# Second MLP of a fused attention and two-MLP kernel: one chunk in eight instead of one in four keeps its second product in fp32

## The reference

```
def _moe2_ref(x, w_in, w_out):
    h = x @ w_in            # 128 -> 2048
    g = h * np.cos(h)
    return (g @ w_out).astype(np.float32)   # 2048 -> 128
```

## Time and profile before

| what | value |
| --- | --- |
| median of 3 runs | 2633.49 us (2632.07 to 2635.88) |
| profiled execution | 2632.91 us |
| its span, first to last instruction | 2631.1 us |
| mean granted TensorE clock | 0.989 of full speed |
| busy over the span: PE, ACT, DVE, POOL | 98%, 92%, 89%, 78% |
| DMA | 17 GB/s mean |

### The profile page before, as it was taken

How to read it: one execution, slowest core, us unless ns; L and a number is a source line. 1 busy time by engine, 2 the same in 40 slices (tenths; PEclk the granted TensorE clock), 3 DMA queues, 4 the chain that set the end, 5 groups by cost and what they waited for, 6 DMA issues and landing times.

```text
span 2631.1 us, 38615 instructions
## 1 busy us (share of the span) xinstructions
PE 2584.3 (98%) x10691; PEld 1794.6 (68%) x10691; DVE 2341.6 (89%) x2730; ACT 2423.3 (92%) x3173; POOL 2052.3 (78%) x1474
## 2 busy tenths in 40 slices
PE   8699999999999999999999999999999999999999
PEld 5366656665666666665656688888888888888887
DVE  4599999999999999999999888888888888888887
ACT  5499999999999999999999899999999999999998
POOL 0189999999999999999999777777777777777776
PEclk9699999999999999999999999999999999999999
DMA  7000000000002000000000000000000000000000
GB/s 220 21 8 11 10 8 11 7 11 7 11 17 71 8 11 7 11 8 11 7 11 5 1 12 12 12 11 11 11 11 11 11 11 11 11 11 11 11 11 15
DMA packets 25688, 45.52 MB, mean 17 GB/s; under 512 B 2888, under 2 KB 11880, under 8 KB 25384
## 3 DMA queue, kind: packets, MB, share of 16 engines
q1 hardware_dynamic: 25640, 44.92, 5.7%
HBM read 16.99 MB, written 12.78 MB: 11 GB/s over the span
## 4 chain that ended last, share of the span: by engine, by line
PE 62%; POOL 14%; issue 10%; DVE 8%; ACT 4%; DMA 1%; POOLq 1%; DVEq 0%; ACTq 0%; SPq 0%
PE bank L1166 22%; PE bank L1158 20%; POOL work L379 8%; PE bank L1016 8%; PE bank L1023 8%; DVE work L776 5%; POOL work L367 3%; POOL part_hi L389 2%; ACT work L532 2%; DVE bank L758 1%; PE bank L947 1%; PE bank L1149 1%; ACT work L520 1%; POOL part_hi L383 1%; DVE work L767 1%
## 5 line engine op out<-in xcount | busy, mean ns | idle before, releaser
L446 POOL TENSOR_TENSOR act_lo<-work,act_hi 128x960 fp32r<-128x960 f32 (+1 forms) x416 | 723.4, 1744 | 330.1 <-ACT act_hi L607 322.1
L1023 PE MATMUL bank<-work,v 128*128 128x480 f32 x1664 | 742.5, 568 | 0.2 <-ACT tokens_t L539 0.2
L1016 PE MATMUL bank<-part_hi,stack_now 96*128 96x480 f32 x2496 | 665.0, 400 | 13.7 <-DVE stack_next L704 7.1
L379 POOL TENSOR_TENSOR work<-work 128x960 f32<-128x960 f32 x278 | 621.9, 2237 | 42.3 <-POOL work L367 3.4
L912 DVE SCALAR_TENSOR_TENSOR work<-work,bank 128x960 f32<-128x960 int32 x416 | 479.6, 1153 | 155.3 <-ACT work L594 155.3
L1016 PEld LDWEIGHTS bank<-part_hi,stack_now 96*128 96x128 f32 x2496 | 434.9, 189 | 241.8 <-DVE work L776 161.9
L758 DVE SCALAR_TENSOR_TENSOR bank<-bank,over_c,work 128x960 f32<-128x960 f32 x416 | 508.4, 1222 | 42.8 <-PE bank L1016 34.1
L776 DVE SCALAR_TENSOR_TENSOR work<-bank,coef_a,work 128x960 f32<-128x960 f32 x416 | 502.2, 1207 | 0.2 <-PE bank L1016 0.2
L515 ACT ACTIVATE work<-work,made 128x960 f32<-128x960 f32 x416 | 469.1, 1128 | 26.2 <-POOL work L379 26.2
L594 ACT ACTIVATE work<-bank 128x960 int32<-128x960 f32 x416 | 404.2, 972 | 93.1 <-PE bank L1158 93.1
L918 DVE TENSOR_TENSOR work<-work,bank 128x960 f32<-128x960 f32 x416 | 477.2, 1147 | 0.0
(11 more groups left out here) (120 smaller groups left out, 3039.3 us busy)
## 6 DMA issues: line engine op xcount, KB each, us to landing
x_group<-tokens_t SPq DMA_DIRECT2D x52, 240.0 KB, 2.2
out_dram<-work SPq DMA_DIRECT2D x52, 240.0 KB, 2.4
x_ring<-in_x_dram SPq DMA_DIRECT2D x40, 240.0 KB, 6.1
work<-in_x_dram SPq DMA_DIRECT2D x12, 240.0 KB, 4.0
stack_now<-stack_next SPq DMA_DIRECT2D x8, 288.0 KB, 3.0
work<-in_moe_w_in_dram SPq DMA_DIRECT2D x1, 1024.0 KB, 15.4
w_raw<-in_moe_w_in_dram SPq DMA_DIRECT2D x1, 1024.0 KB, 4.9
v<-in_moe_w_out_dram SPq DMA_DIRECT2D x2, 0.5 KB, 13.9
```

The lines of the kernel that those rows point to most:

```text
L379: nc.gpsimd.tensor_tensor(quot[k % 3], square[k % 3], abs_h[k % 3], ALU.add).then_inc(den_ready, 1)
L446: nc.gpsimd.tensor_tensor(act2_lo[:, k % 2, w], angle[k % ANGLES][:, w], act2_hi[:, k % 2, w].bitcast(F32), ALU.subtract).then_inc(act2_pa ...
L1016: mm = pe.matmul(place_out[:, t, :], stack_now[:, i, w], part_hi[0:K3, place, :], start=start, stop=stop, skip_group_check=not start)
L1023: mm = pe.matmul(sums, v[:, 2 * u + t, :], g[:, t * GROUP:(t + 1) * GROUP], start=(2 * u + t == 0), stop=(2 * u + t == CHUNKS - 1))
```

## The change

`split_to` gives 480 columns only to every fourth unit (units 3 and 7 of a group) instead of every second (1, 3, 5 and 7). So in units 1 and 5 of each group, 104 units in all, the second chunk goes in parts as well. `part_v2` parts four chunks instead of three for even j, since chunks 3 and 11 are now needed in parts; chunks 7 and 15 stay in fp32.

```diff
         def split_to(k):
 
-            return GROUP if k % 2 else UNIT
+            return GROUP if k % 4 == 3 else UNIT
...
             def part_v2(j):
 
-                c = slice(4 * j, 4 * j + 3)
+                c = slice(4 * j, 4 * j + (4 if j % 2 == 0 else 3))
                 nc.gpsimd.tensor_copy(v2_hi[:, c, :], v2[:, c, :]).then_inc(v2_parted, 1)
                 pool.wait_ge(v2_parted, 2 * j + 1)
                 nc.gpsimd.tensor_tensor(v2_lo[:, c, :], v2[:, c, :], v2_hi[:, c, :].bitcast(F32), ALU.subtract).then_inc(v2_parted, 1)
```

## The result

The changed kernel takes 2636.6 us (median of 20 runs, 2632.87 to 2639.82). The kernel before, run 20 times as well, takes 2631.47 us (2627.01 to 2635.88). The ratio is 1.0021, 95% interval 1.0014 to 1.0027: slower by 5.1 us, at the very edge of what the prediction called no change. The three runs known before it (2633.49) lay 2 us high, so the forecast time of 2636.0 is closer to the measured one than the forecast effect, +2.5 us, is to +5.1: that the times agree to 0.6 us is in part luck.

What follows compares the result with a forecast made beforehand. TensorE was taken to bound the kernel. Per group, 0.30 us saved against a 0.35 us stall behind GpSimd gave 0.05 us longer; 50 groups made 2.5 us, ScalarE and ends nothing: 2636.0 us, 8-in-10 range 2624 to 2646.

Steps and rivals of the forecast that it cites:

- What bounds: From 1700 to 2600 us TensorE is busy throughout and sets the time; no other engine does.
- Rival (d): The fp32 product is hidden, so the change does not do what it says; answered no, no chance stated.
- TensorE's saving: Second products of units 1 and 5: 0.15 us saved per changed unit, 0.30 a group, 15.6 us in all.
- ScalarE at nothing: High parts of units 1 and 5 take 0.40 us more each, covered by wait and spare time, costed at nothing.
- Rival (c): ScalarE becomes second late engine over three full units in a row: 5 us on top, 2641 us; chance 0.15.
- GpSimd: Longer low part of unit 1 delays `low_y` and unit 2's low part; TensorE waits in `end2(2)`, 0.35 us a group.
- The release: From the start of a 960-column low part to TensorE's next work behind its two matmuls: 2.83 us.
- The stall: TensorE's wait in `end2(2)` for unit 2's low part: next first product at 2003.90 instead of 2003.55, 0.35 us.
- The restart: TensorE resuming after the wait for GpSimd: 0.15 us of release and restart, stall bounds 0.20 and 0.54.
- The ends: First and last group, including `part_v2` and the end chain on GpSimd: cancel to within 0.3 us, taken as 0.
- (a): TensorE's gain stays because the low part of unit 2 isn't late: 2618 us; chance 0.15, whole or in half.
- (b): Slower: costlier restart in `end2(2)`; with the full weight load stall 0.54, 12 us, 2646 us; chance 0.2.

Runs made afterwards that it cites:

- run 20: Not a label of a follow-up: the kernel before was run 20 times, like the changed kernel; median 2631.47 us.
- TensorE's part alone: Against the changed kernel, ScalarE and GpSimd keep 480 columns in odd units, TensorE still does six float32r matmuls in units 1 and 5: 2614.2 us, ratio 0.9939.
- unit 1 alone: Against the kernel before, the change made only in unit 1 of each group, unit 5 keeping its fp32 product: 2644.05 us, ratio 1.0055.
- `low_y` elsewhere: The changed kernel with `low_y` issued one step later on GpSimd, behind the low part of unit 2: 2615.05 us, ratio 0.9944 to the kernel before.
- the widened side engines: Against the kernel before, ScalarE and GpSimd make 960 columns in units 1 and 5, TensorE keeps the fp32 product: 2646.98 us, ratio 1.0065.

## Why the prediction was right, and where it was off

What bounds: right. TensorE before; TensorE's part alone shows that taking work off it alone gives all of it back as time. Rival (d) falls with it.

TensorE's saving: 0.15 us a unit forecast, 0.158 to 0.160 measured in two kernels. Four passes at the distance of the float32r matmuls (the Trainium skill, FP8 and Floating Point Precision, TensorE Precision Notes) would have made it 0.21; the measurement decides for the rows.

ScalarE at nothing: right. After, its turns wait 200 times for TensorE, up to 0.3 us each, and the waits for line 918 stay at 8. At the place where the prediction counted on 0.04 us to spare, the high part of unit 1 and the turns of unit 4 now stand like this:

```profile
1995.61 0.99 ACT L607 CAST act_hi<-work 128x960 fp32r<-128x960 f32 x1
1996.57 0.98 ACT L594 ACTIVATE work<-bank 128x960 int32<-128x960 f32 x1
```

That is 0.96 us from start to start, where it was 0.93 before (1996.30 to 1997.23): the cover held to 0.03 us. Rival (c) is out for this change: neither the change in unit 5 alone nor the kernel with fp32 in units 1 and 7 loses anything.

GpSimd: the place, the mechanism and its count (once a group, 50 times) were right, each term a little small. Start to start of a full low part in this place is 2.24 us, not the 2.20 of rows 5, where the next step was the short cast and not `low_y`. The release is 2.85, not 2.83. The stall is 0.40 us in the group shown and 0.43 on the mean (3.03 less 2.60), and the lengths of the group give 0.118 + 2 x 0.159 = 0.44, against 0.35 forecast; in unit 1 alone 0.295 + 0.158 = 0.45. This is the term that was mis-sized, by 0.08 to 0.09 us. The terms above account for 0.06 of it; where the rest comes from is open. Since the net is a difference of two like numbers, 0.44 - 0.32 instead of 0.35 - 0.30, it doubled the effect: 0.118 us a group for 0.05, 5.1 us for 2.5. The point from which the prediction called it slower, 5.3 us, lies between the 5.9 us that the groups give and the 5.1 us of the times.

The restart: between the bounds of the prediction, 0.20 and 0.54, and at the row taken. The load and the matmul are again at the same moment, 2002.73, and the two matmuls take 0.53 us to the next work instead of 0.43. That a matmul can begin before its weight load completes is what the Trainium skill says (TensorE: Matmul & The Clock Gate, Architectural detail); the trace, with both at one start, does not speak against that. It does speak against what the prediction made of it, a restart that costs nothing: 0.1 us is lost, and no run here shows to what.

The ends: taken as 0. The second MLP begins at 1479.81 us in the trace of before and at 1477.23 in that of after, and lasts 1151.3 and 1157.0 us: 5.7 us more, where 50 groups of 0.118 are 5.9. In the last group TensorE now waits twice for low parts, 1.08 and 0.64 us, where it waited once:

```profile
2624.76 0.70 PE L1166 MATMUL bank<-act_lo,v_hi 128*128 128x480 f32 x2 [1.08 <-POOL act_lo L446]
...
2626.96 0.70 PE L1166 MATMUL bank<-act_lo,v_hi 128*128 128x480 f32 x2 [0.64 <-POOL act_lo L446]
```

Of the rivals (a) is what the kernel does with `low_y` elsewhere, 2615.05 us for the 2618 forecast. (b) has the sign and the place, but the stall grew by only half of what it needs, to 0.43 or 0.44 and not to 0.54.

## What to carry to other kernels

An engine that is busy 71% of the stretch, 81% after the change, can set the time: what counts is not its total but whether one wait falls into the slack of its place, so walk one period start by start. Where work is shifted to an engine in order, look at the step queued behind it; the same edit was worth -0.158 us at one unit and +0.295 at another, and one step moved turned a loss of 5 us into a gain of 15. Where the profile names no releaser ("issue"), set the start beside the ends of the other engines: a constant distance gives away a wait. After each fix walk the period again, for the pinch moves: it came back at the next unit, then at the producer that had been moved too late.

## What the runs showed beside that

The part of the kernel ahead of the second MLP has the same code in all these kernels, and yet in the profiled runs its end (the first matmul of `product_in`) lies anywhere from 1473.61 (the widened side engines) to 1480.69 us (TensorE's part alone). That is 7 us, more than the effect of the change; what makes it differ no run shows. Within the second MLP the groups of one trace agree to 0.2 us or better. Where an edit touches one stage that repeats, the length of its period tells apart what the total, in a few runs, can't: the kernel with fp32 in units 1 and 7 is 3 us behind the one with `low_y` moved by its median, and level with it by its group (21.543 and 21.542).
